# GpSimd's gathers of the second mixture, in runs of three to five with weight parts between

## The reference

```python
# attention over chunks of 64 tokens, 4 x 8 heads, head size 64, 576 tokens
attn = softmax(q_c @ k_c.T / 8) @ v_c            # -> x: 2304 tokens x 512
# first mixture: every token goes through all 4 experts
for e in range(4):
    x2 += p[:, e:e+1] * (relu(x @ w1[e]) @ w2[e])        # 512 -> 1024 -> 512
# second mixture: every token goes through one of 8 experts
expert_idx = argmax(x2 @ w_gate)
for e in range(8):
    out[mask_e] = gate_w[mask_e] * (relu(x2[mask_e] @ v1[e]) @ v2[e])
```

## Time and profile before

| what | us |
|---|---|
| three runs, median (lowest, highest) | 1137.49 (1136.7, 1146.06) |
| the profiled execution's own time | 1139.17 |
| its span, first to last instruction | 1137.4 |
| TensorE busy | 1114.6 (98%) |
| VectorE, ScalarE, GpSimd busy | 563.9, 289.4, 312.3 |
| mean granted clock of TensorE | 0.993 |

### The profile page before, as it was taken

How to read it: one execution, slowest core, us unless ns; L and a number is a source line. 1 busy time by engine, 2 the same in 40 slices (tenths; PEclk the granted TensorE clock), 3 DMA queues, 4 the chain that set the end, 5 groups by cost and what they waited for, 6 DMA issues and landing times.

```text
span 1137.4 us, 19057 instructions
## 1 busy us (share of the span) xinstructions
PE 1114.6 (98%) x6750; PEld 976.2 (86%) x6750; DVE 563.9 (50%) x1142; ACT 289.4 (25%) x429; POOL 312.3 (27%) x191
## 2 busy tenths in 40 slices
PE   9999999999999999999999999999999989999995
PEld 6899888999889999988999998889877778888884
DVE  5445434322221232222223248888655358988985
ACT  3444344331111133111113311112242023032220
POOL 7300000250000024000002401100377759168781
PEclk9999999999999999999999999999999989999998
DMA  9332221420000021000002101101672459379996
GB/s 355 79 103 83 74 74 28 150 74 0 0 0 0 0 82 65 0 0 0 0 0 92 56 29 29 21 7 28 186 186 67 136 179 243 63 214 222 211 193 109
DMA packets 104868, 97.71 MB, mean 86 GB/s; under 512 B 64111, under 2 KB 88815, under 8 KB 104690
## 3 DMA queue, kind: packets, MB, share of 16 engines
q1 hardware_dynamic: 81602, 60.23, 21.8%
q10 hardware_dynamic: 18720, 25.22, 7.5%
q0 software_dynamic: 4496, 11.56, 3.4%
HBM read 73.48 MB, written 10.92 MB: 74 GB/s over the span
## 4 chain that ended last, share of the span: by engine, by line
PE 91%; DVE 3%; DMA 2%; another core or an unknown queue 1%; issue 1%; SPq 0%; POOL 0%; ACT 0%; POOLq 0%; DVEq 0%
PE psum L1428 15%; PE psum L1430 14%; PE psum L1429 14%; PE psum L1474 12%; PE psum L1475 11%; PE psum L1476 11%; PE psum L1666 3%; PE psum L1668 3%; PE psum L1667 3%; DMA h_planes_T<-h_planes 1%; PE psum L1356 1%; PE psum L1340 1%; DMA rows<-x_rows,meta 1%; PE psum L1628 1%
## 5 line engine op out<-in xcount | busy, mean ns | idle before, releaser
L476 POOL TENSOR_TENSOR weights_r<-weights,weights_r 128x1024 fp32r<-128x1024 f32 x96 | 233.2, 2451 | 612.9 <-ACT weights_r L666 611.8
L1428 PE MATMUL psum<-xhi,weights_r 128*128 128x384 f32 (+1 forms) x772 | 260.0, 337 | 0.0
L1430 PE MATMUL psum<-xhi,weights_r 128*128 128x384 f32 (+1 forms) x772 | 257.9, 334 | 0.0
L1429 PE MATMUL psum<-xlo,weights_r 128*128 128x384 f32 (+1 forms) x772 | 257.7, 334 | 0.0
L1474 PE MATMUL psum<-weights_r,hhi 128*128 128x512 f32 x576 | 226.9, 394 | 0.0
L1476 PE MATMUL psum<-weights_r,hlo 128*128 128x512 f32 x576 | 224.8, 390 | 0.0
L1475 PE MATMUL psum<-weights_r,hhi 128*128 128x512 f32 x576 | 224.7, 390 | 0.0
L661 ACT ACTIVATE hhi<-psum 128x384 fp32r<-128x384 f32 x192 | 94.5, 492 | 482.5 <-PE psum L1430 482.5
L910 DVE SCALAR_TENSOR_TENSOR hlo<-psum,hhi 128x384 fp32r<-128x384 f32 x192 | 106.4, 556 | 218.1 <-ACT hhi L661 218.1
L666 ACT ACTIVATE weights_r<-weights 128x1024 fp32r<-128x1024 f32 x88 | 92.7, 1058 | 214.2 <-DMA weights<-in_moe_w 196.0
L1428 PEld LDWEIGHTS psum<-xhi,weights_r 128*128 128x128 f32 x772 | 144.9, 188 | 1.7
(11 more groups left out here) (189 smaller groups left out, 1094.6 us busy)
## 6 DMA issues: line engine op xcount, KB each, us to landing
weights<-in_moe_w SPq DMA_DIRECT2D x48, 512.0 KB, 4.6
weights<-in_moe_w ACTq DMA_DIRECT2D x48, 512.0 KB, 5.0
qkT<-in_qk SPq DMA_DIRECT2D x18, 512.0 KB, 4.0
v_rows<-in_v SPq DMA_DIRECT2D x18, 256.0 KB, 3.5
x_rows<-xfin SPq DMA_DIRECT2D x18, 256.0 KB, 5.3
wg_row<-in_gate_rows SPq DMA_DIRECT2D x1, 2048.0 KB, 7.4
h_planes_T<-h_planes SPq DMA_TRANSPOSE x38, 5.1
rows<-x_rows,meta POOLq DMA_INDIRECT x26, 3.7
```

What stands on the lines that cost most here:

```text
L476: gp.tensor_tensor(rounded(set_, 1, c), raw(set_, c), rounded(set_, 0, c).bitcast(F32), ALU.subtract).then_inc(sem("w1_lo" if c < NW // 2 ...
L1428: mm(out_, ahi, bhi, start=(i == 0), stop=False)
L1429: mm(out_, ahi, blo, start=False, stop=False)
L1430: last = mm(out_, alo, bhi, start=False, stop=(i == n - 1))
```

## The change

It changes two tables. The batches from the fifth on are cut in another way, into ten batches in place of nine, and the low parts of place 1's chunks 3 to 7 stand at other places in the row of gathers. The gathers, their order and the splits are the same ones, in the same number.

```diff
-    BATCH = [range(0, 1), range(1, 2), range(2, 4), range(4, 6), range(6, 8), range(8, 10), range(10, 13), range(13, 18),
-             range(18, NB)]
+    BATCH = [range(0, 1), range(1, 2), range(2, 4), range(4, 6), range(6, 8), range(8, 11), range(11, 15), range(15, 19),
+             range(19, 22), range(22, NB)]
     NEAR = 5
     FIRST_TURNED = 6
-    SPLITS = {1: [], 2: [3, 4], 3: [5], 4: [6], 5: [7], 6: [], 7: [], 8: []}
+    SPLITS = {3: [3], 5: [4], 6: [5], 7: [6], 8: [7]}
...
-                split_place(1, SPLITS[n])
+                split_place(1, SPLITS.get(n, []))
```

## The result

In the comparison made with the prediction the changed kernel took 1132.1 us (median of 11 runs, 1128.49 to 1136.19) and the kernel before 1139.78 (median of 11, 1136.7 to 1146.06). The ratio is 0.9934, with a 95% interval of 0.9919 to 0.9948: 7.5 us less, where 0.7% and 7.8 us were predicted. The time of 1132.1 us is 2.4 us above the predicted 1129.7; the kernel before was 2.3 us slower here too than the 1137.49 us from which the prediction started.

What follows compares the result with a forecast made beforehand. TensorE, busy for 98% of the span, was taken to bound the kernel. 1139.17 - 7.8 = 1131.4 us for a profiled execution, with the median 1.7 us lower, gave 1129.7 us, range 1128.1 to 1139.2.

Steps and rivals of the forecast that it cites:

- The stall as the only term: TensorE's block from 901.2 to 921.3 us: its 7.8 us excess goes, everything else costs 0; chance 0.57.
- the rival in which half is left: Same stall: DMA pressure falls by only some 28%, so 3.9 us are gained, 1133.6 us; chance 0.12.
- Gathers in a long run as its cause: GpSimd's unbroken 15 gathers and scatter of XB, from 891.30 us, stall all engines until the run ends; costs 7.8 us.
- The rival in which it belongs to its place in the program: Stall comes from instruction fetching or a message queue, not the gathers' run; time unchanged at 1137.5 us; chance 0.22.
- The rival in which it gets worse: Stall goes by GpSimd's pauseless work, so lasts from about 880 to 907.1 us: 12.0 us more, 1149.5; chance 0.09.
- The nearest rows: Later runs of five and six scatters (953.4, 1035.3 us) leave TensorE fully busy, so the whole 7.8 us is gained.
- Waits and moved low parts at 0: GpSimd's new waits for meta are met, at least 2.5 us ahead; later low parts keep 30 to 40 us cover; cost 0.
- What is late next: Place 2's low parts end about 922.5 us, before first_product(6) at 926.5; 6 to 8 us of cover stay.
- The profiled execution: Whole kernel under the profiler: 1139.17 - 7.8 = 1131.4 us.
- The rule of the Trainium skill: If it is the whole story, gathers cannot hold VectorE or TensorE, the cause is another and the sum is 0.

Runs made afterwards that it cites:

- the kernel that gathers first: Changed kernel with all 24 gathers in one run, then the five low parts, then the scatter of XB: ratio 1.0034 to the kernel before, 1141.05 us.
- the kernels with rows of eight: Changed kernel with only three breaks (ratio 0.9890, 1129.22 us); kernel before with only its low parts moved, old batches kept (0.9885, 1129.61 us).
- the last two comparisons: Kernel before, unedited, rerun beside the changed kernel and both kernels with rows of eight (1130.88 us), then once more for its profile (1130.68 us).
- the kernel with half rows: Kernel before with each gather of blocks 10 to 24 as two indirect DMAs of 1024 bytes per row: ratio 1.0174, 1161.7 us.
- the low parts early: Changed kernel's new batches with the low parts back at their old places, 15 DMAs unbroken: ratio 0.9983 to the kernel before, 1137.34 us.

## Why the prediction was right

**The stall as the only term.** Right. The excess of one block was put at 7.8 us and all of it went; the ratio gives 7.5. The median by itself would not have shown it: 1132.1 us is nearer to the 1133.6 of the rival in which half is left than to 1129.7. The ratio decides (the interval of 0.9919 to 0.9948 holds the forecast of 0.993 and not the 0.9966 of that rival), and the four blocks in the profile. GpSimd's row came out as worked out: g8 at 875.09 (874.9), the last batch at 902.50 (903), the scatter's end at 907.46 (907.1).

**Gathers in a long run as its cause.** Shown, where the stall occurs: it came back with the long run (0.9983), moved with it, grew with its length (28.7 us), and went with breaks of 2.4 us or more between runs of up to eight, filled or idle. Through what the run holds the other engines isn't shown. The rival in which it belongs to its place in the program falls with the kernel that gathers first. The rival in which half is left was half right in kind: VectorE was late by 1.0 and 0.7 us in the run of five, but TensorE had cover. The rival in which it gets worse falls: GpSimd worked without a pause above 1.0 us from 862.82 to 907.46 and TensorE never stopped, so work of GpSimd as such doesn't bring the stall.

**The nearest rows.** I took the gain because runs of five and six scatters left TensorE alone. That held, and the kernels with rows of eight show a margin above it.

**Waits and moved low parts at 0.** Right. No new wait shows in GpSimd's timeline, and the low parts of place 1 had their cover.

**What is late next.** Right with a smaller margin: place 2's low parts ended at 924.6, not 922.5, because the first loads took 5.95 us to ScalarE's first high part (908.01 to 913.96) where they had taken 3.94 (914.47 to 918.41); now they fall into the last gathers. The last low part is needed by the second half of first_product(6), 2.7 us behind its begin: at 929.3 now (926.64 + 2.7) and at 937.0 before (934.26 + 2.7). So the cover went from 8.0 us (937.0 - 929.0) to 4.7 (929.3 - 924.6), and it sufficed.

**The profiled execution.** It was put at 1131.4 and took 1132.95. The 1.6 us were lost at the very end and not at the gathers: TensorE's last wait, for VectorE's hTlo, ends at 1107.41 where it ended at 1115.15, 7.7 us sooner, but from there on it took 23.8 us and not 22.3. The stretches from that wait to the end, changed kernel and kernel before:

```profile
1107.40:1131.20 23.80, 14.06 (x48) 11.03 (x48) 9.40 (x12) 0.00 (x0) 3.11 (x4) 0.72 0.62 98
```
```profile
1115.10:1137.40 22.30, 13.04 (x48) 10.02 (x48) 9.46 (x12) 0.00 (x0) 3.56 (x4) 0.82 0.61 104
```

The same 48 matmuls, at a mean granted clock of 0.72 instead of 0.82, take 1.0 of the 1.5 us. The runs of the changed kernel differ by up to 7.7 us from each other, so this is no more than their spread.

**What the prediction didn't have.** It held the stall for a fixed cost of the kernel. In the last two comparisons the kernel before was at 1130.9 and 1130.7 us by itself; in the one with the changed kernel beside it the ratio is 0.9991, with an interval that holds 1. That the forecast was put to the test where the stall occurs was luck: the reasoning gave no ground for it, and in the later comparisons a gain of 0.7% would have been wrong. A second profile of the same kernel, taken at another time, could have shown it.

## What to carry to other kernels

When several engines stand still at once, between instructions that have no wait, and start again within 0.03 us of each other, look at what one other engine issues meanwhile: here a row of a dozen and more indirect DMAs on GpSimd, 1.30 us apart, whose number and not whose bytes did it. Here it was enough to break such a row every three to five with 2.4 us of work that GpSimd had to do anyway; a memset of 0.12 us was no break, and idle ones were paid for by TensorE, which waited 3.0 us for GpSimd next. And profile a kernel more than once, at different times, before a stall without a releaser is taken for a part of it: this one came and went on the same chip with the same program.

## What the runs showed of the hardware

- In the stall TensorE, VectorE and ScalarE are late together, and GpSimd isn't: TensorE starts a single matmul each 2.1 or 2.8 us in the kernel with half rows, VectorE's take_result comes 6.5 us late in the kernel before and 12.4 in the one with half rows (914.99, behind a product that ended at about 902.6), ScalarE needs 29.0 us for 17 issues in the kernel that gathers first and 17.5 in the kernel before, while GpSimd's DMAs stay 1.30 us apart and land, as far as it is on record, in 3.3 to 4.1 us. The starts of TensorE stand 0.70 us or a multiple of it apart (919.20, 921.30, 923.40, 926.20). Why is not shown.
- The rule of the Trainium skill that stood against the reading (page "SBUF — State Buffer", section "Who interferes with whom": only the pair of ports of VectorE and GpSimd is contended, and TensorE and ScalarE wait for nobody) doesn't explain the stall, since TensorE and ScalarE were held as well. The rule speaks of SBUF ports; that they have a part here no run shows, and none rules it out for VectorE.
- TensorE's first gap comes 15 to 16 us, or 12 to 13 DMAs, into the run in five kernels. In the one that gathers first it comes 21 us behind the first gather, but 12 us and ten DMAs behind a pause of 1.55 us in the row (872.39). In the five it was at nearly the same place of TensorE's program, so this is no clean measure of an onset. VectorE was late as early as the fifth DMA of a run (878.17 in the changed kernel).
- The idle time also costs clock: from 911.9 to 917.7 the matmuls run at the lower level, 0.50. The mean over the disturbed block was 0.83 in the kernel before, 0.91 with the low parts early and 0.62 with half rows.
